# Block 0 of windowed attention pair by pair, its sinks unit by unit, and the first front product between the last units

## What is computed

```python
# q, k, v: (2, 8, 768, 64); n_sink = 4, window = 128
scores = scale * np.matmul(q, k.transpose(0, 1, 3, 2))
keep = is_sink | in_window          # key < 4, or 0 <= query - key < 128
a = softmax(where(keep, scores, -1e9));  attn = a @ v
x = attn.transpose(0, 2, 1, 3).reshape(1536, 512)
x = (silu(x @ w_gate) * (x @ w_val)) @ w_out          # 512 -> 1536 -> 512
h = x @ w_in;  out = (max(h, 0) + alpha * min(h, 0)) @ w_out2   # 512 -> 2048 -> 512
```

## Time and profile before

| | |
|---|---|
| median of three runs | 633.64 us (633.48 to 634.05) |
| the profiled execution | 634.69 us, its span 633.0 us |
| PE busy | 622.8 us, 98% of the span |
| DVE, ACT, POOL busy | 409.9, 244.6, 453.5 us |
| the chain that ended last | 94% PE, 3% DVE, 1% ACT |

### The profile page before, as it was taken

How to read it: one execution, slowest core, us unless ns; L and a number is a source line. 1 busy time by engine, 2 the same in 40 slices (tenths; PEclk the granted TensorE clock), 3 DMA queues, 4 the chain that set the end, 5 groups by cost and what they waited for, 6 DMA issues and landing times.

```text
span 633.0 us, 9382 instructions
## 1 busy us (share of the span) xinstructions
PE 622.8 (98%) x3072; PEld 489.1 (77%) x3072; DVE 409.9 (65%) x696; ACT 244.6 (39%) x585; POOL 453.5 (72%) x600
## 2 busy tenths in 40 slices
PE   8889999999999999999999999999999999999997
PEld 5467776777777888888887888887788888888886
DVE  4954566666486966564747474898786567756474
ACT  4736554545535532121212030445534424442150
POOL 6848778787778989998989674689999887810000
PEclk9999999999999999999999999999999999999999
DMA  9343333321222011221212322100212222000004
GB/s 292 121 151 101 123 89 124 118 68 51 71 81 84 34 35 53 68 74 40 68 33 67 99 78 57 39 13 17 68 66 67 68 67 84 17 1 0 2 17 183
DMA packets 29391, 45.67 MB, mean 72 GB/s; under 512 B 2880, under 2 KB 9024, under 8 KB 29344
## 3 DMA queue, kind: packets, MB, share of 16 engines
q1 hardware_dynamic: 29200, 44.81, 22.5%
q10 hardware_dynamic: 144, 0.26, 0.1%
HBM read 41.92 MB, written 3.15 MB: 71 GB/s over the span
## 4 chain that ended last, share of the span: by engine, by line
PE 94%; DVE 3%; ACT 1%; issue 1%; DVEq 0%; ACTq 0%
PE ffn_ps L1987 29%; PE att_ps L1962 24%; PE ffn_ps L1902 15%; PE att_ps L1987 8%; PE ffn_ps L1962 6%; PE att_ps L1849 3%; PE att_ps L1811 2%; PE att_ps L1828 2%; DVE scratch L2214 1%; PE att_ps L1994 1%; PE att_ps L1902 1%; PE att_ps L1859 1%; PE ffn_ps L1849 1%; PE att_ps L1803 0%; PE att_ps L1805 0%
## 5 line engine op out<-in xcount | busy, mean ns | idle before, releaser
L1672 POOL TENSOR_TENSOR w_lo<-raw_weights,w_hi 128x512 fp32r<-128x512 f32 (+1 forms) x128 | 155.7, 1216 | 10.3
L1671 POOL CAST w_hi<-raw_weights 128x512 fp32r<-128x512 f32 (+1 forms) x128 | 80.1, 625 | 30.7 <-PE ffn_ps L1987 17.1
L2331 DVE TENSOR_TENSOR scratch<-ffn_ps,scratch 128x512 f32<-128x512 f32 x108 | 74.0, 687 | 34.6 <-PE ffn_ps L1987 34.1
L1700 POOL TENSOR_TENSOR w_lo<-part_sum,w_hi 128x256 fp32r<-128x256 f32 x80 | 59.8, 748 | 6.4
L1902 PE MATMUL ffn_ps<-x_hi,w_hi 128*128 128x512 f32 x152 | 61.6, 405 | 0.7 <-DVE x_lo L2240 0.6
L1902 PE MATMUL ffn_ps<-x_hi,w_lo 128*128 128x512 f32 x152 | 59.4, 391 | 0.0
L1902 PE MATMUL ffn_ps<-x_lo,w_hi 128*128 128x512 f32 x152 | 59.3, 390 | 0.0
L1752 POOL TENSOR_TENSOR scratch<-scratch,inv 128x264 f32<-128x264 f32 (+1 forms) x48 | 30.0, 626 | 31.6 <-DVE inv L2203 31.3
L1987 PE MATMUL ffn_ps<-h_hi,w_hi 128*128 128x512 f32 x130 | 51.5, 396 | 0.0
L1987 PE MATMUL ffn_ps<-h_hi,w_lo 128*128 128x512 f32 x130 | 50.7, 390 | 0.0
L1987 PE MATMUL ffn_ps<-h_lo,w_hi 128*128 128x512 f32 x130 | 50.6, 389 | 0.0
(11 more groups left out here) (210 smaller groups left out, 1581.2 us busy)
## 6 DMA issues: line engine op xcount, KB each, us to landing
raw_weights<-pieces SPq DMA_DIRECT2D x122, 256.0 KB, 2.7
k_sb<-kt SPq DMA_DIRECT2D x12, 264.0 KB, 3.5
v_sb<-vt SPq DMA_DIRECT2D x12, 256.0 KB, 2.7
out<-scratch SPq DMA_DIRECT2D x12, 256.0 KB, 2.0
q_sb<-qt SPq DMA_DIRECT2D x11, 256.0 KB, 3.5
scratch<-vs SPq DMA_DIRECT2D x1, 384.0 KB, 5.6
q_sb<-qt ACTq DMA_DIRECT2D x1, 256.0 KB, 2.4
alpha<-alpha_t SPq DMA_DIRECT2D x1, 8.0 KB, 6.5
```

The costliest lines, as they stand in the source:

```text
L1671: chain(pool.tensor_copy(hi, raw[:, r % n_raw, at]))
L1672: last = pool.tensor_tensor(lo, raw[:, r % n_raw, at], hi.bitcast(F32), ALU.subtract)
L1700: pool.tensor_tensor(lo, s, hi.bitcast(F32), ALU.subtract).then_inc(split_done, 1)
L2331: ins = dve.tensor_tensor(to, back_ps(key), total, ALU.add)
```

## The change

In block 0 the unit `u` is no longer tile `u // 4`, pair `u % 4`. The pair is the outer loop, and its tiles go in the order 1, 2, 3, 0. The inputs of the first four tiles are laid out pair by pair in memory for that, so that one DMA brings all four tiles of a pair. Keys carry their sinks behind instead of ahead, and in a tile that has a previous one a score product is 264 columns wide instead of 260.

In block 0 the sinks go with their unit: the 8 sink columns of the two heads lie side by side in `p_sb`, PE transposes them as a third transpose (L1860 of the kernel after), ACT copies the 8x128 result to `pts_head` (`copy_sinks`, L2083), and PE adds one product (L1890) between the halves of the unit's values. The gather, the two DVE instructions and the four products for tiles 1 to 3 are gone. Tiles from 4 on keep them.

With a pair complete after four units, `x_hi` and `x_lo` hold a quarter of the features for the whole block. The first front product is cut in four by features (`begin`): the first quarter goes between values(13) and turn(15), the second and the third behind values(15), the fourth in the chunk itself after scores(16). The dummy products ahead of turn(14) are gone, and turn goes ahead of values in one more slot.

```diff
+    HEAD_TILES = (1, 2, 3, 0)
+    def place(u):
+        return (HEAD_TILES[u % quads_t], u // quads_t) if u < early else divmod(u, n_pairs)
...
+    first_g = groups_b[0]
+    begun = {(first_g, 0, 0): n_k - 1}
     for w in range(early + LAG):
         item = slot(w, 0, early)
...
+        if w == early:
+            plan.append(("begin", (first_g, 0, 0, 0)))
...
+    plan += [("begin", (first_g, 0, 0, kk)) for kk in range(1, n_k - 1)]
     emit_slot(slot(early, early, n_units))
...
+            def load_head(g):
+                sp.dma_start(k_sb[:, g, :, :], kt[g]).then_inc(k_in[g], 16)
+                if g:
+                    sp.dma_start(q_sb[:, g, :, :], qt[g]).then_inc(q_in[g], 16)
+                sp.dma_start(v_sb[:, g, :, :], vt[g]).then_inc(v_in[g], 16)
             def load_keys(c):
                 r = c % RING
+                for done in scores_done:
+                    sp.wait_ge(done, max(early, scores_until(c - RING + 1)))
...
             def load_values(c):
+                for done in pv_done:
+                    sp.wait_ge(done, max(early, scores_until(c - RING + 1)))
...
-                if n_slot in (1, 2, early, early + 1):
+                if n_slot in (early - 4, early - 3, early, early + 1):
                     split_v_sink(sinks_split // 2, sinks_split % 2)
...
             def scores(u):
-                        last = pe.matmul(ps[:, 0:2 * P + n_sink], q, both[:, n_sink:], start=True, stop=True)
+                        last = pe.matmul(ps[:, 0:2 * cols], q, both, start=True, stop=True)
...
-            fills = {0: 2, 1: 4, 2: 2, early - 2: 2}
+            fills = {0: 2, 1: 4, 2: 2}
             def turn(u):
...
+                if head_sinks(u):
+                    last = pe.transpose(turn_ps(u)[0:2 * n_sink, block_cols(2)], p_sb[:, u % 8, P:P + 2 * n_sink], ident[:, :])
...
             def values(u):
...
+                    if m == 0 and head_sinks(u):
+                        if u == 0:
+                            pe.wait_ge(head_sink_in, 16)
+                        pe.wait_ge(head_sink_done, head_sinks_until(u))
+                        pe.matmul(x, v_sink_head[:, block_cols(g)], pts_head[:, block_cols(u % 2)],
+                                  start=False, stop=False, skip_group_check=True)
...
+            def front_products(g, f, part, kk):
...
+                awaited = g == first_g and part == 0 and f == 0
+                if awaited:
+                    pe.wait_ge(xhi_done, kk + 1)
+                passes = ((0, 0), (1, 0), (0, 1)) if awaited else PASSES
+                for a, b in passes:
+                    if awaited and b == 1:
+                        pe.wait_ge(xlo_done, kk + 1)
+                    last = pe.matmul(ps, w_parts[a][:, block_cols(kk)], x_parts(kk)[b],
...
+            def begin_front(g, f, part, kk):
+                if kk == 0:
+                    pe.wait_ge(split_done, job_no["piece", piece_key(g, f, part, single)])
+                    pe.wait_ge(exp_done, 2 * early)
+                front_products(g, f, part, kk)
...
-                    if n[3] == early - 2:
+                    if n[3] in (early - 3, early - 2):
                         turn(n[2])
                         values(n[3])
...
+            def copy_sinks(u):
+                act.wait_ge(pt_done, u + 1)
+                if u >= 2:
+                    for done in pv_done:
+                        act.wait_ge(done, u - 1)
+                act.activation(pts_head[:, block_cols(u % 2)], turn_ps(u)[0:2 * n_sink, block_cols(2)],
+                               ACT.Copy).then_inc(head_sink_done, 1)
...
             for what, n in plan:
+                if what == "slot":
+                    if n[3] is not None and head_sinks(n[3]):
+                        copy_sinks(n[3])
+                    if n[0] is not None:
+                        exps(n[0])
```

More of the change, by code:

```diff
@@ L1518, in has_prev, with stacked_sinks, sinks_until, head_sinks @@
             return tile(c) > 0
[L1520 to L1526, removed]
+        def stacked_sinks(s):
+            return s >= quads_t and has_prev(s)
+        def sinks_until(s):
+            return sum(stacked_sinks(e) for e in range(s + 1))
+        def head_sinks(u):
+            return u < early and has_prev(place(u)[0])
+        def head_sinks_until(u):
+            return sum(head_sinks(v) for v in range(u + 1))
         event_at = {event: n for n, event in enumerate(plan)}
@@ L1897, in front @@
                                                   and event_at["back", key] < event_at["front", (g, f, part, 0)]))
-                ps = front_ps(g, f, part)
-                w_parts = piece(g, f, part, single)
-                for kk in range(half * half_k, (half + 1) * half_k):
-                    for a, b in PASSES:
-                        last = pe.matmul(ps, w_parts[a][:, block_cols(kk)], x_parts(kk)[b],
-                                         start=kk == 0 and (a, b) == (0, 0),
-                                         stop=kk == n_k - 1 and (a, b) == (1, 0))
+                for kk in range(max(done, half * half_k), (half + 1) * half_k):
+                    last = front_products(g, f, part, kk)
                 if half == 1:
@@ L2041, in round_x @@
                 if c < quads_t:
[L2042 to L2043 removed]
+                    act.activation(x_hi[:, c, :], bank(home(c, quads_t), 3), ACT.Copy).then_inc(xhi_done, 1)
                 else:
@@ L2147, in _ @@
             for what, n in plan:
-                if what == "slot" and n[0] is not None:
-                    exps(n[0])
+                if what == "slot":
[3 more added lines that the diff above has]
+                        exps(n[0])
                 elif what == "x":
@@ L2192, in taken_until @@
             def taken_until(u):
-                return sum(2 if tile(v // n_pairs) == 1 else 1 for v in range(u + 1))
+                return sum(2 if tile(place(v)[0]) == 1 else 1 for v in range(u + 1))
             def maximum(u):
-                at = n_sink if not has_prev(u // n_pairs) else 0
+                at = n_sink if not has_prev(place(u)[0]) else 0
                 dve.wait_ge(taken, taken_until(u))
-                dve.tensor_reduce(top[:, u % 4, :], score_ps(u)[:, :, P + at:2 * P + n_sink],
+                scores = both_heads(u, cols, cols) if not at else score_ps(u)[:, :, cols:cols + P]
+                dve.tensor_reduce(top[:, u % 4, :], scores,
                                   mybir.AxisListType.X, ALU.max).then_inc(top_done, 1)
```

211 lines of the change are left out of this document (107 added, 104 removed).

## The result

| | before | after |
|---|---|---|
| median (lowest to highest), us | 633.68 (633.08 to 634.68), 6 runs | 654.90 (650.91 to 655.59), 6 runs |
| profiled execution: time, span | 634.69, 633.0 | 650.91, 649.2 |
| mean granted clock of its runs | 0.949 in the profiled one | 0.979 in the profiled one, 0.969 to 0.971 in the five others |

The change costs 21.2 us: ratio 1.0321 (95% interval 1.0294 to 1.0347). The forecast was 639.9, range 636.2 to 642.3. The sign was right and the size was not: the result lies 12.6 above the range.

The account below looks back on a forecast made before the run. PE was taken as the bound, with the head's ring of waits moving all that follows. Terms +1.0 + 2.75 + 1.55 + 1.55 + 1.25 - 2.2 + 0.3 = +6.2 on 633.64 gave 639.9, range 636.2 to 642.3; dear ends +9.0.

Parts of the forecast that it names:

- rival 4: Head of the kernel: PE's new waits throw its clock back for some 4 us of work, +3, 643; chance 0.03.
- ACT's copy: ScalarE's 8x128 copy of a unit's sinks in block 0: 0.30, cheap end 0.20, dear end 0.36.
- The sink product: PE's added float32 product per unit with sinks, two instructions: 0.29 together, cheap end 0.15, dear end 0.38.
- The third transpose: PE's added transpose of a unit's 8 sink columns: 0.20, cheap end 0.07.
- One pair: Four units in steady state in block 0: 9.73 against 8.18, +1.55 for each of two middle pairs.
- the ring: Head's wait cycle: DVE spread, PE values, next transposes, next spread; one turn 1.91, lengthened by steps put between spreads.
- Start and first pair: First spread moves by +1.0; the first pair then takes 10.4 against 7.63, +2.75.
- Last pair: From unit 12's spread to unit 15's: 6.1 against 4.85, +1.25.
- The end, -2.2: From the last spread to the thirteenth front product: 3.9 against 6.07, the change's gain.
- Late weights (rival 3): After the head: late weight pieces hold POOL, PE waits for units 16 and 17; 641 to 642, chance 0.10.
- Later: PE after the head: 28 units have 16 more columns in four instructions, +0.3; nothing else changes on PE.
- Rivals 1 and 2: Block 0: 1, sinks' steps hide in PE's waits, 631.3, chance 0.05; 2, products nearly free, copy still waits, 634.7, chance 0.07.

Follow-up runs that it names:

- the filled kernel: Changed kernel with products of zeros in PE's two waits (spread, ScalarE's copy) of units 4, 8 and 12: 643.73, ratio 1.0159.
- the second trace: The changed kernel once more, unaltered, traced in one run: 653.07, mean clock 0.971.
- the sink product last: Changed kernel with zero products in PE's waits, sink product behind all values, x_hi rounding behind ScalarE's sink copy: 640.47, ratio 1.0107.
- the sooner weights: Weight pieces 6 to 9 loaded ahead of the late keys and values, added to the 640.47 kernel: 639.35, ratio 1.0081.

## Why the prediction was right and wrong

**The step that failed is rival 4, the clock, for which the sum has no term.** It was seen: "PE now stands still some 1 us once in each pair, and half as long once more". It was given 0.03 and sized at "some 4 us of PE work, +3". It happened in every run and lasted 27 us in one trace and about 38 in the other. It cost 11.2 by the medians (654.90 against 643.73 with the waits filled); the run with the 27 us lies only 7.2 over the filled kernel. The argument against it, "the granted clock of the head is 0.96 with 5.9 of waits in it", was the fault: it took a mean over 42 us for evidence on two waits close together, 1.34 us in all. (In that execution the column reads 0.95 from 8 us to the end, at full pace; see the last section.) PE had only four values instructions between 0.58 and 0.76 of standing still. The trace of before has no such place: its longest wait, 0.78, has only 0.23 ahead of it. And nothing in the profile of before said how long a fall lasts; +3 was a guess in the form of a sum.

That is not all. With the clock held the change still costs 10.1, over the range and over the dear end of +9.0. Two terms of the sum were too small, the sink product and the late weights; both are below.

**Prices.**
- *ACT's copy*: 0.25, forecast 0.30 (0.20 to 0.36). Right.
- *The sink product*: 0.41 from its start to the next (22.96 to 23.37), forecast 0.29 and dear end 0.38. Too low: 12 x 0.12 = 1.4. I had priced an instruction by the stacked products, which run in one pass of another type; the two float32 instructions have 0.2 each. Leaving the twelve out gave 0.36 each. That its eight rows don't make it cheap was right: 8x384 and 96x384 both last 0.91.
- *The third transpose*: 24.22 - 24.02 = 0.20, as taken.

**One pair**: +1.86 for +1.55 (10.04). The steps are 3.39 (20.94 to 24.33) for 3.29, then 2.48 for 2.33, 2.53 for 2.54 and 1.64 for 1.57. The mechanism of the ring was right; with the sink product at 0.41 the first two would have come out at 3.41 and 2.45, and only the third too long, at 2.66.

**Start and first pair**: 10.00, so +0.44 for +1.0, and 9.44 in the second trace, so -0.12; then 20.94 - 10.00 = 10.94, +3.31 for +2.75. Together 3.75, as summed, by luck: two errors cancel.

**Last pair**: 47.66 - 41.09 = 6.57 in the kernel with filled waits, +1.7 for +1.25.

**The end, -2.2**: in the same kernel 51.97 - 47.66 = 4.31 against 6.07, so -1.8. The size was about right, and the reason, the early front, was mostly wrong. Without it the stretch is no longer than 4.81 (45.41 to 50.22), so it makes 0.5 of the 1.8. The rest comes with the order: the last unit has no sinks and three pairs' x is ready, which is argued from the order and was not taken apart. Where the two were measured side by side, the early front gave 0.1.

**Late weights (rival 3)**: in the changed kernel hidden (0.28), by the fall of the clock. With the clock held it cost 1.1 to 1.6 beside the sink product last, where the wait was 1.31, and more with the filled waits alone, where it was 2.08. The prediction took nothing for it, and up to 1 in the range.

**Later**: 587.8 for 588.5 + 0.3; the +0.3 didn't show.

**The sum.** 13th with waits filled at 51.97: +7.5. The terms ahead of "later" gave +5.9. The difference of 1.6 is about the sink product's 1.4; start and first pair err on both sides. What follows it in that trace is 2.6 longer than before (the wait of 2.08 and the slow products behind it, which by their mean clock two of the four runs have). So the medians give 10.1 in place of 6.2 for everything but the fall, and 11.2 for the fall. That 11.2 is a net price, since the fall hides the late weights. Rivals 1 and 2 are out: PE waits for the copy, the order without sinks' steps costs nothing, and the sink products are not nearly free.

## What to carry to other kernels

When a change makes TensorE stand still twice close together in a stretch of short products, price a fall of its clock by the whole stretch up to the next dense products and some 8 us of these, not by the wait: here 1.3 us of waits cost 11 us. Single waits of up to 0.92 us did no such harm. Look for it in the column of the granted clock and in an instruction's own length, since busy shares rise when it happens. Shortening one of the waits by moving a step (a copy ahead of a longer rounding, a product behind the values) did more than filling them (637.0 against 643.73, of which the sooner weights are 1.1 to 1.6), and filling one of three places did nothing. Price a product by a row of the same type and number of passes; and before crediting an early start, count which of its instructions fill waits and which only change places.

## What the hardware showed that I had not expected

- **A long fall lasted into the front products.** At 0.50 PE was busy 23.63 of 24.00 (36 to 60) and 31.41 of 32.00 (28 to 60). In all three traces with a long fall the clock came back 8 to 9 us behind the first front product, wherever it had fallen (first products at 52.35, 54.16 and 58.46; clock back at about 60.4, 62.9 and 67.7, worked out from the mean clock of the stretches). The two short falls, one less than 2 us ahead of the first front product (38.02) and one among front products (behind the wait of 2.08), were over in under 4 us.
- **At the lower level nothing takes quite twice as long.** Four values instructions last 0.69 for 0.44, a 512-column front product comes every 0.43 for 0.23; a pair took 14.76 for 10.04. Where PE waits for others anyway, 16 us at the slow pace cost 2.5.
- **The granted clock as shown is not always comparable.** In the profiled execution before it reads 0.95 from 8 us to the end; after it reads 1.00 where the clock has not fallen; and the front products come every 0.23 in both. Without its products of zeros the kernel before reads 1.00 from 8 to 20 us, while instructions last as long as at 0.50 (eight values instructions 1.12 in both):

```profile
8.00:20.00 12.00, 11.53 (x54) 5.46 (x52) 8.10 (x24) 7.08 (x36) 10.04 (x18) 1.00 0.74 250
```

  So the length of a known instruction is the check on that column, above all at the start.
